# The order of the eighteen products of a step in the expert stage, a different one in each of the four experts

## The chip, the cores and the metric

The kernel runs on one core of a Trainium2 chip. The metric is the device time of one execution in microseconds (us), as a median of several runs. Beside it stands one execution that the hardware profiler recorded.

## The reference, cut to what matters

```python
def _attn_ref(q, k, v, alpha):                 # gated linear attention, state per head
    for t in range(S):
        state = alpha[:, :, t, :, None] * state + np.einsum('bhd,bhe->bhde', k[:, :, t], v[:, :, t])
        y[:, :, t] = np.einsum('bhd,bhde->bhe', q[:, :, t], state)

def _moe_ref(x, w1, w2, w3, w_out):
    a = x @ w1
    b = x @ w2
    h = a * b @ w3
    return h @ w_out

def _moe2_ref(x, domain_probs, w1, w2):        # N 3072 tokens, D 384, E 4 experts, F 1024
    p = domain_probs / (domain_probs.sum(-1, keepdims=True) + 1e-09)
    for e in range(E):
        h = np.maximum(x @ w1[e], 0.0)
        out += p[:, e:e + 1] * (h @ w2[e])
```

The three run one after the other. The change lies in the last one, the four experts.

## The kernel before

Up to about 414 us the kernel computes the attention and the bilinear layer (`up1`, `down1`, products of 384 columns, three split terms each through `split_product`, lines 1061 to 1063). From there on TensorE works on the experts. Tokens are on the columns: 3072 tokens are six tiles of 512, taken two at a time in a round, so three rounds for each expert. F is eight blocks of 128 rows. A step is one block of one tile; a round has sixteen steps (`STEPS2`), steps 0 to 7 on its first tile (u = 0) and 8 to 15 on its second (u = 1).

A step has two halves of nine matrix products each. Every number is split into a high and a low part, so each product of matrices takes three terms (high by high, high by low, low by high), over three blocks of 128 (`KT`).
- U (up, `up2_product`, line 1220): x1 times the expert's first weights, nine products of 128x512 that add up in one PSUM bank, `bank[s % 2]`.
- D (down, `down2_product`, line 1337): h times the expert's second weights. Products 0 to 2 add into a first bank, 3 to 5 into a second, 6 to 8 into a third (`SUM_BANKS[u]`, banks 5, 6, 7 for u = 0, the first two of which the profile calls score_banks, and 2, 3, 4 for u = 1).

`step2(e, m, s, ahead)` waits until the low part of h of step s is ready (`h_lo_ready`), and then issues the nine D of step s and the nine U of step s + 2 in turns: D, U, D, U, and so on. The U of step s + 2 end with a signal (`up_done`), on which h of that step is made on the other engines while TensorE works on step s + 1. In expert 0 this is `h_high` on ScalarE and `h_low` on VectorE. In experts 1 to 3 it is a chain of three: VectorE applies the ReLU and the gate (`scaled_low`, line 1030, out of PSUM into `h_scaled`), ScalarE makes the high part (`scaled_high`, line 726), VectorE the low part (line 1033). After the last step of a tile VectorE adds the three sums to `total` (`add`, lines 1019 to 1023), for which it waits on `down_done`. The last two steps of the last expert have nothing ahead, so they are nine D each. Two of the three rounds of an expert run in a hardware loop, the third is written out.

What makes some U products different is two sets at the top of the file, which `up2_product` looks up by expert, step and product number:

```python
BY_TURNS = {(e, s, i): run for e, run in enumerate((4, 2, 8)) for s, i in ((1, 0), (FT + 1, 4))}
IN_HALVES = {(EXPERTS - 1, s, i) for s, i in ((1, 1), (FT + 1, 4))}
```

A product in `BY_TURNS` computes the same sum in another order of its 512 columns: it takes a run of 4 (2, 8) columns from the first half, then as many from the second half, and so on, in what it reads and in what it writes. A product in `IN_HALVES` is issued as two instructions of 256 columns. Each of these stands twice in every round: at a product of step 1 and of step 9. The text below calls both of them odd products. Expert 0 has odd products with runs of 4, expert 1 of 2, expert 2 of 8, expert 3 the halves. Before the experts' loop, `up2(0, 0, 0)` and `up2(0, 0, 1)` issue nine U each with no D between them, the second with an odd product in front.

Of the kernel before, what the change touches and what calls it, by code (L numbers as in the profile page):

```python
# [26 lines left out]
ALU = mybir.AluOpType  # L27
ACT = mybir.ActivationFunctionType
# [3 lines left out]
BATCH, HEADS, SEQ, D = 4, 8, 768, 48  # L32
# [10 lines left out]
DM, FF, EXPERTS = 384, 1024, 4  # L43
KT, FT = DM // P, FF // P
# [9 lines left out]
TILE2 = 512  # L54
TILES2 = TOKENS // TILE2
STEPS2 = 2 * FT
ROUNDS = TILES2 // 2
# [6 lines left out]
BEGUN_BY_ACT = 2  # L64
FOLD_BANKS = [0, 1, 2, 3, 4, 0, 1, 2]
SUM_BANKS = [[5, 6, 7], [2, 3, 4]]
BY_TURNS = {(e, s, i): run for e, run in enumerate((4, 2, 8)) for s, i in ((1, 0), (FT + 1, 4))}
IN_HALVES = {(EXPERTS - 1, s, i) for s, i in ((1, 1), (FT + 1, 4))}
TERMS = 3
WARM = 6  # L70
CONSTANTS = 7
# [17 lines left out]
def gated_attention_experts(nc, akq, v, akq_long, v_columns, w3T, w_out, wsets, probs, out):  # L89
# [5 lines left out]
    with ExitStack() as ctx:  # L95
        def sb(name, shape, dt=F32, where=ctx):
            return where.enter_context(nc.sbuf_tensor(name, shape, dt))

        def sem(name):
            return ctx.enter_context(nc.semaphore(name))  # L100

        bank = [ctx.enter_context(nc.psum_tensor(f"bank{i}", [P, 512], F32)) for i in range(5)]
# [11 lines left out]
        h_hi = sb("h_hi", [P, 2, TILE2], F32R)  # L114
        h_lo = sb("h_lo", [P, 2, TILE2], F32R)
# [52 lines left out]
        we_raw, we_hi, we_lo, x1_hi, x1_lo = [None, None], [None, None], [None, None], [None, None], [None, None]  # L168
# [18 lines left out]
        gate_rows = [sb(f"gate_rows{i}", [P, TOKENS]) for i in range(2)]  # L187
        h_scaled = sb("h_scaled", [P, 2, TILE2])
# [83 lines left out]
        h_scaled_ready = sem("h_scaled_ready")  # L272
        h_hi_ready = sem("h_hi_ready")
        h_lo_ready = sem("h_lo_ready")
# [36 lines left out]
        def chunk_beside(b, s, last_batch):  # L311
            t, i = divmod(s, FT)
            if i >= 2 * CHUNKS1 or (t == 1 and last_batch):
                return None
            return (b, CHUNKS1 + i // 2) if t == 0 else (b + 1, i // 2)

        def chunk_behind(b, c, count=1):

            n = CHUNKS * b + c + count
            return divmod(n, CHUNKS) if n < BATCH * CHUNKS else None  # L320
# [175 lines left out]
        def _(pool):  # L496
# [30 lines left out]
            def bilinear(b, beside=True, last_batch=False):  # L527
                for s in range(STEPS1):
                    chunk = chunk_beside(b, s, last_batch) if beside else None
                    if chunk and s % 2 and chunk_behind(*chunk, 2):  # L530
                        scale_queries(*chunk_behind(*chunk, 2))
                    if s + 1 < STEPS1 or (beside and not last_batch):
                        g_low(b, s + 1)
                    if last_batch and beside and FT <= s < FT + PIECES // 2:
                        pieces_low(1, s - FT)
                    if last_batch and beside and s == FLAG_STEP:
                        pool.wait_ge(flag_ready, 2)
                        flag = pool.value_load(regular[:, :], min_val=0, max_val=1)
                return flag if last_batch and beside else None
# [20 lines left out]
        def _(act):  # L560
# [161 lines left out]
                h_high(0, 0)  # L722

            def scaled_high(e, m, s):
                act.wait_ge(h_scaled_ready, STEPS2 * ((e - 1) * ROUNDS + m) + s + 1)
                act.activation(h_hi[:, s % 2, :], h_scaled[:, s % 2, :], ACT.Copy).then_inc(h_hi_ready, 1)  # L726

            def step_high(e, m, s):
                if e == 0:
# [21 lines left out]
        def _(dve):  # L751
# [234 lines left out]
            with dve.If(is_regular == 0):  # L986
                dve.sem_inc(redo_value_free, 1)
                dve.sem_inc(redo_y_ready, 1)
                with dve.Fori(0, BATCH) as b:
# [13 lines left out]
                    for c in range(CHUNKS):  # L1003
                        dve.wait_ge(redo_turned, CHUNKS * b + c + 1)
                        t, i = divmod(c, CHUNKS1)
# [18 lines left out]

            def scaled_low(e, m, s):
                n = e * ROUNDS + m
                at = bass.ds((2 * m + s // FT) * TILE2, TILE2)
                dve.wait_ge(gate_rows_loaded[e % 2], 16 * (e // 2 + 1))
                dve.wait_ge(up_done, STEPS2 * n + s + 1)
                dve.scalar_tensor_tensor(out=h_scaled[:, s % 2, :], in0=bank[s % 2][:, :], scalar=0.0, in1=gate_rows[e % 2][:, at],  # L1030
                                         op0=ALU.max, op1=ALU.mult).then_inc(h_scaled_ready, 1)
                dve.wait_ge(h_hi_ready, STEPS2 * n + s + 1)
                dve.tensor_tensor(h_lo[:, s % 2, :], h_scaled[:, s % 2, :], h_hi[:, s % 2, :], ALU.subtract).then_inc(h_lo_ready, 1)  # L1033

            def step_low(e, m, s):
                if e == 0:
# [21 lines left out]
        def _(pe):  # L1058
            def split_product(dst, left, right, first, last):

                pe.matmul(dst, left[0], right[0], start=first, stop=False)  # L1061
                pe.matmul(dst, left[0], right[1], start=False, stop=False)  # L1062
                return pe.matmul(dst, left[1], right[0], start=False, stop=last)  # L1063
# [138 lines left out]
            def up2_waits(e, m, s):  # L1202
                u, f = divmod(s, FT)
                if f == 0:
                    pe.wait_ge(x1_loaded[u], 32 * (e * ROUNDS + m + 1))
                    if u == 0 and isinstance(m, int) and m == 0:
                        pe.wait_ge(piece_lo, PIECES * (e + 2))

            def up2_product(e, s, i):

                u, f = divmod(s, FT)
                k, term = divmod(i, TERMS)
                cols = slice(k * FF + f * P, k * FF + (f + 1) * P)
                parts = [(bank[s % 2][:, :], (x1_lo if term == 1 else x1_hi)[u][:, k, :])]
                if (e, s, i) in BY_TURNS:
                    parts = [tuple(a.rearrange("p (h a r) -> p a h r", h=2, r=BY_TURNS[e, s, i]) for a in part) for part in parts]
                if (e, s, i) in IN_HALVES:
                    parts = [tuple(a[:, half:half + TILE2 // 2] for a in parts[0]) for half in (0, TILE2 // 2)]
                for dst, moving in parts:
                    mm = pe.matmul(dst, (we_hi if term < 2 else we_lo)[e % 2][:, cols], moving, start=(i == 0), stop=(i == KT * TERMS - 1))  # L1220
                if i == KT * TERMS - 1:
                    mm.then_inc(up_done, 1)

# [35 lines left out]
            for k in range(FT):  # L1259
# [5 lines left out]
                for f in range(FOLD_FIRST):  # L1265
                    if (k, f) == (0, 1):
                        pe.wait_ge(w3_loaded[0], 16)
                    cols = slice(f * P, (f + 1) * P)
                    if k < SPLIT_FROM:
                        mm = pe.matmul(bank[FOLD_BANKS[f]][:, 0:DM], w3_sb[:, k, cols], wo_sb[:, k, :], start=(k == 0), stop=False)  # L1270
                    else:
                        i = k - SPLIT_FROM
                        mm = split_product(bank[FOLD_BANKS[f]][:, 0:DM], (w3_hi[:, i, cols], w3_lo[:, k, cols]),
                                           (wo_hi[:, i, :], wo_lo[:, i, :]), False, k == FT - 1)
# [7 lines left out]
            for n in range((FT - FOLD_FIRST) * FT):  # L1282
                f, k = FOLD_FIRST + n // FT, n % FT
# [4 lines left out]
                mm = pe.matmul(bank[FOLD_BANKS[f]][:, 0:DM], w3_sb[:, k, f * P:(f + 1) * P], wo_sb[:, k, :], start=(k == 0), stop=(k == FT - 1))  # L1288
# [14 lines left out]
            with nc.body("redo_products", valid_engines=[pe.engine]):  # L1303
                with pe.Fori(0, BATCH) as b:
                    with pe.Fori(0, REDO_ROWS) as i:
                        pe.wait_ge(redo_product_ready, REDO_ROWS * b + i + 1)
                        for c in range(CHUNKS):
                            mm = pe.matmul(bank[5][:, 2 * c:2 * c + 2], redo_product[:, c * CHUNK:(c + 1) * CHUNK], head_sum[:, :],
                                           start=True, stop=True)
                        mm.then_inc(redo_summed, 1)  # L1310
                    for c in range(CHUNKS):
# [3 lines left out]
                        for k in range(KT):  # L1315
                            mm = pe.transpose(bank[7][:, k * P:(k + 1) * P], y_sb[:, k * P:(k + 1) * P], identity[:, :])
# [11 lines left out]
            def down2_product(e, m, s, i):  # L1328

                u, f = divmod(s, FT)  # L1330
                part, term = divmod(i, TERMS)
                if term == 0 and f == 0:
                    if e == 0 and u == 1 and part == 0:
                        pe.wait_ge(x1_lo_ready, X1_LOW_AHEAD + KT * TILES1 * BATCH)
                    pe.wait_ge(added, KT * (e * TILES2 + 2 * m + u) + part + 1)
                cols = slice(KT * FF + f * DM + part * P, KT * FF + f * DM + (part + 1) * P)
                mm = pe.matmul(bank[SUM_BANKS[u][part]][:, :], (we_hi if term < 2 else we_lo)[e % 2][:, cols], (h_lo if term == 1 else h_hi)[:, s % 2, :],  # L1337
                               start=(f == 0 and term == 0), stop=(f == FT - 1 and term == TERMS - 1))
                if f == FT - 1 and term == TERMS - 1:
                    mm.then_inc(down_done, 1)  # L1340

            def step2(e, m, s, ahead):

                pe.wait_ge(h_lo_ready, STEPS2 * (e * ROUNDS + m) + s + 1)
                if ahead:
                    up2_waits(*ahead)
                for i in range(KT * TERMS):
                    down2_product(e, m, s, i)
                    if ahead:
                        up2_product(ahead[0], ahead[2], i)  # L1350

            def round2(e, m, following):

# [69 lines left out]
```

## Time and profile before

| | us |
|---|---|
| median of 3 runs | 1217.36 (1217.21 to 1217.63) |
| the profiled execution | 1217.92 |
| its span, first to last instruction | 1216.2 |
| TensorE matmul busy, of the span | 1210.0 (99%) |
| TensorE weight load busy | 1039.6 (85%) |
| VectorE busy | 549.2 (45%) |
| ScalarE busy | 287.1 (24%) |
| GpSimd busy | 161.2 (13%) |

The span is 1.7 us shorter than the time of the same execution. A matmul of 512 columns is shown with a length of about 0.39 us, but the next one starts 0.23 us after it: they overlap. The length of one therefore says little; what counts is the distance from one start to the next, called pitch below. The timeline gives starts to 0.01 us, so a pitch is read over many products. A view of stretches counts in "(x...)" also the product that is still running at the start of the stretch; where a stretch begins at the start of a product, the number of pitches in it is one less than that count.

### The profile page before, as it was taken

What the parts mean: (1) busy time and instruction counts of PE and PEld (TensorE: products, weight loads), DVE (VectorE), ACT (ScalarE), POOL (GpSimd) and SP (SyncE); (2) the same over time, 40 slices, a digit from 0 to 9 for tenths busy, and PEclk for the clock granted to TensorE, in tenths of its full rate; (3) what the DMA queues carried; (4) which work ended last, traced back from release to release, by engine and by line L of the source; (5) the groups of instructions that cost most, each with busy time, mean ns of one, the idle gap of its engine ahead of it and who ended that gap; (6) DMA issues with size and microseconds to landing.
All of it is one profiled execution on the core that took longest, in us unless ns stands there. A gap on an engine that the chain in (4) does not pass through costs nothing.

```text
span 1216.2 us, 17647 instructions
## 1 busy us (share of the span) xinstructions
PE 1210.0 (99%) x7170; PEld 1039.6 (85%) x7170; DVE 549.2 (45%) x1006; ACT 287.1 (24%) x526; POOL 161.2 (13%) x147
## 2 busy tenths in 40 slices
PE   9999999999999999999999999999999999999998
PEld 8799999999999988888888888888888888888887
DVE  6997586686651122122233433333343343443433
ACT  3443333333333311111111121121121111111111
POOL 1132222222223400000000000000000000000000
PEclk9999999999999999999999999999999999999999
DMA  9744544544515361101151111114101111222201
GB/s 282 212 122 113 136 130 106 140 126 98 136 47 188 105 259 52 36 19 49 52 207 53 52 52 52 52 63 197 36 19 49 52 52 52 78 78 78 78 7 46
DMA packets 89782, 114.34 MB, mean 94 GB/s; under 512 B 39152, under 2 KB 57968, under 8 KB 88688
## 3 DMA queue, kind: packets, MB, share of 16 engines
q1 hardware_dynamic: 89424, 112.97, 29.5%
q8 instruction: 49, 0.80, 0.3%
q10 hardware_dynamic: 288, 0.39, 0.1%
q14 instruction: 21, 0.17, 0.0%
HBM read 92.59 MB, written 18.40 MB: 91 GB/s over the span
## 4 chain that ended last, share of the span: by engine, by line
PE 98%; DVE 1%; DMA 1%; ACT 0%; SPq 0%; issue 0%; DVEq 0%; ACTq 0%
PE bank L1220 33%; PE bank L1337 22%; PE score_banks L1337 11%; PE bank L1061 9%; PE bank L1063 9%; PE bank L1062 9%; PE bank L1102 2%; PE bank L1288 1%; PE score_banks L1123 1%; PE bank L1112 1%; PE score_banks L1086 1%; DMA wo_sb<-w_out 1%; DVE total L1023 0%; PE bank L1070 0%; DVE w_lo L918 0%; DVE suffix L762 0%
## 5 line engine op out<-in xcount | busy, mean ns | idle before, releaser
L1220 PE MATMUL bank<-x_lo,we_hi 128*128 128x512 f32 x582 | 226.4, 391 | 0.0
L1220 PE MATMUL bank<-x_hi,we_hi 128*128 128x512 f32 x576 | 226.3, 393 | 0.0
L1220 PE MATMUL bank<-x_hi,we_lo 128*128 128x512 f32 x576 | 225.9, 392 | 0.0
L1030 DVE SCALAR_TENSOR_TENSOR h_scaled<-bank,gate_rows 128x512 f32<-128x512 f32 x144 | 99.4, 690 | 253.9 <-PE bank L1220 253.8
L726 ACT ACTIVATE h_hi<-h_scaled 128x512 fp32r<-128x512 f32 x144 | 91.0, 632 | 494.3 <-DVE h_scaled L1030 494.3
L1337 PE MATMUL bank<-h_hi,we_hi 128*128 128x512 f32 x384 | 150.9, 393 | 0.2 <-DVE h_lo L1033 0.2
L1337 PE MATMUL bank<-h_lo,we_hi 128*128 128x512 f32 x384 | 150.8, 393 | 0.0
L1337 PE MATMUL bank<-h_hi,we_lo 128*128 128x512 f32 x384 | 150.7, 392 | 0.0
L1033 DVE TENSOR_TENSOR h_lo<-h_scaled,h_hi 128x512 fp32r<-128x512 f32 x144 | 99.7, 693 | 100.6 <-ACT h_hi L726 100.6
L513 POOL TENSOR_TENSOR we_lo<-we_raw,we_hi (+1 forms) x48 | 60.9, 1292 | 545.2 <-ACT we_hi L574 545.2
L1220 PEld LDWEIGHTS bank<-x_lo,we_hi 128*128 128x128 f32 x582 | 109.3, 188 | 24.8
L1220 PEld LDWEIGHTS bank<-x_hi,we_lo 128*128 128x128 f32 x576 | 108.2, 188 | 24.5
L1220 PEld LDWEIGHTS bank<-x_hi,we_hi 128*128 128x128 f32 x576 | 108.1, 188 | 24.2
L1061 PE MATMUL bank<-x,wb_hi 128*128 128x384 f32 x384 | 128.6, 335 | 0.0
L1063 PE MATMUL bank<-x,wb_lo 128*128 128x384 f32 x384 | 128.4, 334 | 0.0
L1062 PE MATMUL bank<-x,wb_hi 128*128 128x384 f32 x384 | 128.3, 334 | 0.0
L843 DVE SCALAR_TENSOR_TENSOR h_lo<-bank,h_hi 128x512 fp32r<-128x512 f32 x48 | 33.2, 692 | 146.8 <-ACT h_hi L613 146.5
L524 POOL TENSOR_TENSOR g_lo<-g_sb,g_hi 128x384 fp32r<-128x384 f32 x64 | 66.3, 1036 | 221.2 <-ACT g_hi L603 221.1
L1337 PEld LDWEIGHTS bank<-h_hi,we_hi 128*128 128x128 f32 x384 | 72.2, 188 | 16.9 <-DVE h_lo L1033 0.6
L1337 PEld LDWEIGHTS bank<-h_lo,we_hi 128*128 128x128 f32 x384 | 72.2, 188 | 16.3
L1337 PEld LDWEIGHTS bank<-h_hi,we_lo 128*128 128x128 f32 x384 | 72.2, 188 | 16.2
L833 DVE TENSOR_TENSOR g_sb<-a_sb,bank 128x384 f32<-128x384 f32 x64 | 35.3, 552 | 110.8 <-PE bank L1063 110.8
(103 smaller groups left out, 1657.5 us busy)
## 6 DMA issues: line engine op xcount, KB each, us to landing
x_hi<-x_hi_spill SPq DMA_DIRECT2D x24, 768.0 KB, 4.9
x_lo<-x_lo_spill SPq DMA_DIRECT2D x24, 768.0 KB, 6.4
we_raw<-wset SPq DMA_DIRECT2D x4, 3072.0 KB, 10.6
inputs<-akq SPq DMA_DIRECT2D x24, 448.0 KB, 5.0
values<-v_rows SPq DMA_DIRECT2D x24, 256.0 KB, 3.5
gate_rows<-gate_spill SPq DMA_DIRECT2D x4, 1536.0 KB, 13.7
inputs<-akq SPq DMA_DIRECT2D x24, 224.0 KB, 3.3
x_hi_spill<-x_hi_out SPq DMA_DIRECT2D x8, 576.0 KB, 4.2
```

Of the source, the lines that this page charges most:

```text
L513: pool.tensor_tensor(set_lo(n)[:, at], set_raw(n)[:, at], set_hi(n)[:, at], ALU.subtract).then_inc(piece_lo, 1)
L524: pool.tensor_tensor(g_lo[:, s % 2, :], g_sb[:, s % 2, :], g_hi[:, s % 2, :], ALU.subtract).then_inc(g_lo_ready, 1)
L726: act.activation(h_hi[:, s % 2, :], h_scaled[:, s % 2, :], ACT.Copy).then_inc(h_hi_ready, 1)
L833: dve.tensor_tensor(g_sb[:, s % 2, :], a_sb[:, s % 2, :], bank[1][:, 0:TILE1], ALU.mult).then_inc(g_ready, 1)
L843: dve.scalar_tensor_tensor(out=h_lo[:, s % 2, :], in0=bank[s % 2][:, :], scalar=0.0, in1=h_hi[:, s % 2, :], op0=ALU.max, op1=ALU.subtract) ...
L1030: dve.scalar_tensor_tensor(out=h_scaled[:, s % 2, :], in0=bank[s % 2][:, :], scalar=0.0, in1=gate_rows[e % 2][:, at], op0=ALU.max, op1=ALU ...
L1033: dve.tensor_tensor(h_lo[:, s % 2, :], h_scaled[:, s % 2, :], h_hi[:, s % 2, :], ALU.subtract).then_inc(h_lo_ready, 1)
L1061: pe.matmul(dst, left[0], right[0], start=first, stop=False)
L1062: pe.matmul(dst, left[0], right[1], start=False, stop=False)
L1063: return pe.matmul(dst, left[1], right[0], start=False, stop=last)
L1220: mm = pe.matmul(dst, (we_hi if term < 2 else we_lo)[e % 2][:, cols], moving, start=(i == 0), stop=(i == KT * TERMS - 1))
L1337: mm = pe.matmul(bank[SUM_BANKS[u][part]][:, :], (we_hi if term < 2 else we_lo)[e % 2][:, cols], (h_lo if term == 1 else h_hi)[:, s % 2, : ...
```

## The change

The U and D of a step are issued in an order that the expert's number picks from `ORDERS`: expert 0 in turns as before, expert 1 three D and three U, three times, expert 2 two and two (the last pair in turns), expert 3 nine D and then nine U. Each order begins with a D and ends with a U. `IN_HALVES` is gone, and `BY_TURNS` has the same entries for all experts: product 4 of steps 3 and 9, with runs of 4. In the very last step of the kernel, h is made in two halves of 256 columns on VectorE and ScalarE.

```diff
-BY_TURNS = {(e, s, i): run for e, run in enumerate((4, 2, 8)) for s, i in ((1, 0), (FT + 1, 4))}
-IN_HALVES = {(EXPERTS - 1, s, i) for s, i in ((1, 1), (FT + 1, 4))}
+ORDERS = [9 * "DU", 3 * ("DDD" + "UUU"), 4 * "DDUU" + "DU", 9 * "D" + 9 * "U"]
+BY_TURNS = {(e, s, 4): 4 for e in range(EXPERTS) for s in (3, FT + 1)}
...
+        def h_parts(e, m, s):
+            last = isinstance(m, int) and (e, m, s) == (EXPERTS - 1, ROUNDS - 1, STEPS2 - 1)
+            return [slice(0, TILE2 // 2), slice(TILE2 // 2, TILE2)] if last else [slice(0, TILE2)]
...
             def scaled_high(e, m, s):
-                act.wait_ge(h_scaled_ready, STEPS2 * ((e - 1) * ROUNDS + m) + s + 1)
-                act.activation(h_hi[:, s % 2, :], h_scaled[:, s % 2, :], ACT.Copy).then_inc(h_hi_ready, 1)
+                for i, at in enumerate(h_parts(e, m, s)):
+                    act.wait_ge(h_scaled_ready, STEPS2 * ((e - 1) * ROUNDS + m) + s + 1 + i)
+                    act.activation(h_hi[:, s % 2, at], h_scaled[:, s % 2, at], ACT.Copy).then_inc(h_hi_ready, 1)
...
             def scaled_low(e, m, s):
                 n = e * ROUNDS + m
-                at = bass.ds((2 * m + s // FT) * TILE2, TILE2)
                 dve.wait_ge(gate_rows_loaded[e % 2], 16 * (e // 2 + 1))
                 dve.wait_ge(up_done, STEPS2 * n + s + 1)
-                dve.scalar_tensor_tensor(out=h_scaled[:, s % 2, :], in0=bank[s % 2][:, :], scalar=0.0, in1=gate_rows[e % 2][:, at],
-                                         op0=ALU.max, op1=ALU.mult).then_inc(h_scaled_ready, 1)
-                dve.wait_ge(h_hi_ready, STEPS2 * n + s + 1)
-                dve.tensor_tensor(h_lo[:, s % 2, :], h_scaled[:, s % 2, :], h_hi[:, s % 2, :], ALU.subtract).then_inc(h_lo_ready, 1)
+                for part in h_parts(e, m, s):
+                    at = bass.ds((2 * m + s // FT) * TILE2 + part.start, part.stop - part.start)
+                    dve.scalar_tensor_tensor(out=h_scaled[:, s % 2, part], in0=bank[s % 2][:, part], scalar=0.0, in1=gate_rows[e % 2][:, at],
+                                             op0=ALU.max, op1=ALU.mult).then_inc(h_scaled_ready, 1)
+                for i, part in enumerate(h_parts(e, m, s)):
+                    dve.wait_ge(h_hi_ready, STEPS2 * n + s + 1 + i)
+                    dve.tensor_tensor(h_lo[:, s % 2, part], h_scaled[:, s % 2, part], h_hi[:, s % 2, part], ALU.subtract).then_inc(h_lo_ready, 1)
...
-                parts = [(bank[s % 2][:, :], (x1_lo if term == 1 else x1_hi)[u][:, k, :])]
+                dst, moving = bank[s % 2][:, :], (x1_lo if term == 1 else x1_hi)[u][:, k, :]
                 if (e, s, i) in BY_TURNS:
-                    parts = [tuple(a.rearrange("p (h a r) -> p a h r", h=2, r=BY_TURNS[e, s, i]) for a in part) for part in parts]
-                if (e, s, i) in IN_HALVES:
-                    parts = [tuple(a[:, half:half + TILE2 // 2] for a in parts[0]) for half in (0, TILE2 // 2)]
-                for dst, moving in parts:
-                    mm = pe.matmul(dst, (we_hi if term < 2 else we_lo)[e % 2][:, cols], moving, start=(i == 0), stop=(i == KT * TERMS - 1))
+                    dst, moving = [a.rearrange("p (h a r) -> p a h r", h=2, r=BY_TURNS[e, s, i]) for a in (dst, moving)]
+                mm = pe.matmul(dst, (we_hi if term < 2 else we_lo)[e % 2][:, cols], moving, start=(i == 0), stop=(i == KT * TERMS - 1))
...
             def step2(e, m, s, ahead):
 
-                pe.wait_ge(h_lo_ready, STEPS2 * (e * ROUNDS + m) + s + 1)
+                pe.wait_ge(h_lo_ready, STEPS2 * (e * ROUNDS + m) + s + len(h_parts(e, m, s)))
                 if ahead:
                     up2_waits(*ahead)
-                for i in range(KT * TERMS):
-                    down2_product(e, m, s, i)
-                    if ahead:
-                        up2_product(ahead[0], ahead[2], i)
+                ups = downs = 0
+                for product in ORDERS[e]:
+                    if product == "D":
+                        down2_product(e, m, s, downs)
+                        downs += 1
+                    elif ahead:
+                        up2_product(ahead[0], ahead[2], ups)
+                        ups += 1
```

## Rows read from the trace of the kernel before

**Rows 1.** The page's TensorE clock in 40 slices, and TensorE's waits from 420 us on.
```profile
PEclk9999999999999999999999999999999999999999
...
engine line waited for: us in total, times, longest us
PE bank L1337 <- DVE h_lo L1033: 0.2, 1, 0.2
```
**Rows 2.** Stretches: TensorE busy (x products), clock, DMA share, GB/s; expert 0 to 3.
```profile
420.32:615.54 195.22, 195.22 (x847) 1.00 0.23 83
615.54:814.90 199.36, 199.36 (x865) 1.00 0.20 72
814.90:1014.16 199.26, 199.26 (x867) 1.00 0.20 72
1014.16:1208.17 194.01, 194.01 (x850) 1.00 0.16 56
```
**Rows 3.** The same view, two stretches of expert 0 with no odd product inside.
```profile
421.49:451.35 29.86, 29.86 (x129) 1.00 0.78 297
485.24:517.90 32.66, 32.66 (x143) 1.00 0.14 46
```
**Rows 4.** Timeline: two odd products of expert 0, and where the 0.230 pitch begins.
```profile
451.58 0.42 PE L1220 MATMUL bank<-x_lo,we_hi 128*128 128x512 f32 x1
...
453.23 0.39 PE L1337 MATMUL bank<-h_hi,we_lo 128*128 128x512 f32 x1
...
482.90 0.41 PE L1220 MATMUL bank<-x_hi,we_hi 128*128 128x512 f32 x1
...
485.01 0.39 PE L1337 MATMUL bank<-h_hi,we_lo 128*128 128x512 f32 x1
```
**Rows 5.** Timeline: first and last of nine U (odd product in front of the second nine).
```profile
414.12 0.39 PE L1220 MATMUL bank<-x_hi,we_hi 128*128 128x512 f32 x1
...
415.98 0.40 PE L1220 MATMUL bank<-x_hi,we_lo 128*128 128x512 f32 x1
...
418.02 0.40 PE L1220 MATMUL bank<-x_lo,we_hi 128*128 128x512 f32 x1
...
419.65 0.40 PE L1220 MATMUL bank<-x_hi,we_lo 128*128 128x512 f32 x1
```
**Rows 6.** Timeline: fifteen products of 384 columns, three or nine in a bank.
```profile
300.13 0.33 PE L1063 MATMUL bank<-g_hi,wp_lo 128*128 128x384 f32 x1
...
302.56 0.33 PE L1062 MATMUL bank<-x,wb_hi 128*128 128x384 f32 x1
```
**Rows 7.** Timeline: the last two steps, nine D each, with the chain between.
```profile
1208.17 0.39 PE L1337 MATMUL bank<-h_hi,we_hi 128*128 128x512 f32 x1
...
1208.44 0.69 DVE L1030 SCALAR_TENSOR_TENSOR h_scaled<-bank,gate_rows 128x512 f32<-128x512 f32 x1 [2.06 <-PE bank L1220]
...
1209.16 0.63 ACT L726 ACTIVATE h_hi<-h_scaled 128x512 fp32r<-128x512 f32 x1 [3.51 <-DVE h_scaled L1030]
...
1209.83 0.69 DVE L1033 TENSOR_TENSOR h_lo<-h_scaled,h_hi 128x512 fp32r<-128x512 f32 x1 [0.70 <-ACT h_hi L726]
...
1210.01 0.39 PE L1337 MATMUL bank<-h_hi,we_lo 128*128 128x512 f32 x1
...
1210.57 0.50 PE L1337 MATMUL bank<-h_hi,we_hi 128*128 128x512 f32 x1 [0.18 <-DVE h_lo L1033]
...
1210.91 0.40 PE L1337 MATMUL bank<-h_lo,we_hi 128*128 128x512 f32 x1
...
1212.55 0.39 PE L1337 MATMUL bank<-h_hi,we_lo 128*128 128x512 f32 x1
```
**Rows 8.** Groups by shape: the nearest shorter operations of VectorE and ScalarE.
```profile
L798 DVE TENSOR_TENSOR scores<-score_banks,causal 64x256 f32<-64x256 f32 x24 | 10.3, 428 | 0.3
...
L603 ACT ACTIVATE g_hi<-g_sb 128x384 fp32r<-128x384 f32 x64 | 33.6, 526 | 122.0 <-DVE g_sb L833 122.0
```
**Rows 9.** Timeline of VectorE in a usual step of expert 3: one step's two operations.
```profile
1030.25 0.69 DVE L1030 SCALAR_TENSOR_TENSOR h_scaled<-bank,gate_rows 128x512 f32<-128x512 f32 x1 [2.06 <-PE bank L1220]
1031.64 0.69 DVE L1033 TENSOR_TENSOR h_lo<-h_scaled,h_hi 128x512 fp32r<-128x512 f32 x1 [0.70 <-ACT h_hi L726]
```

## The prediction

> **What bounds the kernel now.** I read the clock first, then TensorE's waits, then stretches of the expert stage, then single products. The granted clock is full in all forty slices, which is the 2.4 GHz level, and from 420 us on TensorE waits once, for 0.2 us, just before the last nine products [rows 1]. So the expert stage is one unbroken stream of products, and its time is their number times the pitch. No other engine and no DMA is on the path until the end.
>
> The pitch is not one number. In the first stretch of expert 0 it is 29.86 / 128 = 0.2333 us, in a later one 32.66 / 142 = 0.2300 us [rows 3]. Both are D and U in turns, with the same shapes, banks and weights. What lies between them is one odd product at 451.58: seven pitches later, at 453.23, the short pitch begins and stays [rows 4]. The stream thus has at least two settled rhythms, 0.2300 and 0.2333, and the start of the stage finds the long one. The reader is to see in the four experts' stretches that the short one then holds to the end: the excess over 0.2300 times the number of 512-column products is 195.22 - 846 x 0.2300 = 0.64 us in expert 0, 199.36 - 864 x 0.2300 = 0.64 in expert 1, 199.26 - 866 x 0.2300 = 0.08 in expert 2, and 194.01 - 843 x 0.2300 = 0.12 in expert 3, whose 849 pitches hold six products in two halves [rows 2]. The sum is 1.48 us.
>
> **The odd products.** Where the stream is already in the short rhythm, an odd product with runs of 4 costs 2.11 us over nine pitches instead of 2.07, so 0.04 us [rows 4]. Before, 0.43 us of expert 0's excess is its long rhythm up to 451.58 (about 134 pitches by 0.0033), the rest its odd products. After, expert 0 has the first odd product with a D between its neighbours at product 4 of step 3, which is issued beside step 1, some 27 pitches from the start instead of 134. That leaves 27 x 0.0033 = 0.09 us of long rhythm, 0.04 for the product, and 5 x 0.04 = 0.20 for the other five, so 0.33 us instead of 0.64. If experts 1 to 3 stayed in the short rhythm, they would pay 18 x 0.04 = 0.72 us instead of 0.64 + 0.08 + 0.12 = 0.84. This part alone brings 0.31 + 0.12 = 0.43 us.
>
> **The last step in halves.** Before, VectorE starts the last h at 1208.44, ScalarE at 1209.16, VectorE again at 1209.83, and TensorE goes on at 1210.57, 0.56 us after the product before it, where 0.23 was due [rows 7]. The chain is 0.69 + 0.63 + 0.69 plus gaps of about 0.03. In halves, a VectorE operation of 256 columns is nearest to the row of 0.43 us; for ScalarE 384 columns take 0.53 and 512 take 0.63, so 256 about 0.42, an estimate by the difference [rows 7, 8]. The first half of the high part starts 0.46 us into the chain, the second ends 0.46 + 0.42 + 0.03 + 0.42 = 1.33, and the second low part ends at about 1.33 + 0.03 + 0.43 = 1.79, since VectorE is done with its first low part by then. Before it was 2.08. That is 0.3 us less of the 0.33 us stall. The longer first pitch behind the wait (0.34 instead of 0.23 [rows 7]) stays if TensorE still arrives first; bounds 0 (each half costs as much as a whole) and 0.44 (stall and longer pitch both gone), taken 0.30. Behind it, the last nine D, the adds and the store are as before.
>
> **The orders, as far as waits go.** Every order begins with D and ends with U, so `up_done` of the step ahead comes at the end of the same eighteen products as before. The chain on it starts at 1030.25 and ends at 1032.33 [rows 9], while TensorE has 18 x 0.23 = 4.14 us of the step between to do. About 2 us of cover stand behind it, and no order takes from that. `down_done` of the third sum comes earlier in the three new orders (in nine and nine after 9 of 18 products instead of 17), so the adds end earlier. In nine and nine the three waits on `added` are three products apart instead of six, but they ask for adds a whole tile back, 8 steps or 33 us. Nothing is queued behind them on TensorE that was not due anyway. Loads of x1 hang on `up_done` as before. I cost this at nothing; if the cover were gone, each late step would show as a wait of TensorE on h_lo.
>
> **The orders, as far as the pitch goes.** This decides. The new orders put products of the same kind behind each other: 12 of 18 pitches in expert 1, 8 of 18 in expert 2, 16 of 18 in expert 3. With 48 steps (46 with something ahead in expert 3) that is 576 + 384 + 736 = 1696 pitches, half from U to U, half from D to D, 848 each. Rows for such pitches are few. U to U: (415.98 - 414.12) / 8 = 0.2325 and (419.65 - 418.02) / 7 = 0.2329, both long, though the first nine came out of a stream without any wait and the second had an odd product in front [rows 5]. D to D: (1210.01 - 1208.17) / 8 = 0.2300 out of the short rhythm, and (1212.55 - 1210.91) / 7 = 0.2343 after the wait [rows 7]. Against an effect of the kind speaks the stream of 384 columns, where products follow in one bank three or nine at a time: (302.56 - 300.13) / 14 = 0.1736 with no sign of a second rhythm [rows 6]. I take 0.0025 us for each U to U and the middle of the D rows, (0 + 0.0043) / 2, cut to 0.0015 since the first of the two is the nearer case (it runs out of the short rhythm, as these will). The sum is 848 x 0.0025 + 848 x 0.0015 = 2.12 + 1.27 = 3.39 us. The pitches between kinds stay at 0.2300. A stream that is not in the short rhythm pays less for an odd product: seven pitches from 451.58 take 1.65 us instead of 7 x 0.2333 = 1.63, so 0.02 and not 0.04 [rows 4]; with 18 of them about 0.4 us less.
>
> The sum against the profiled execution: 1217.92 - 0.43 - 0.30 + 3.39 - 0.36 = 1220.2. Against the median of the runs, which is 0.56 us under the profiled execution, it is 1217.36 + 2.30 = 1219.7. That is the forecast.
>
> A rule against all this. At one column in a cycle of the 2.4 GHz level, 512 columns would take 0.2133 us, and the short rhythm has 0.2300 [rows 3], so 0.0167 us a product are something else; if that something were the change of bank, the new orders would save it. The Trainium skill, TensorE: Matmul & The Clock Gate, section "Back-to-back issue gap", gives N / 2.4 + 2.5 ns, 215.8 ns for 512 columns, and the same page, "A second HAM failure mode", says that cycling through PSUM banks makes TensorE idle for moments. By these the pitch could come down towards 0.216; the trace doesn't agree where it has products in one bank [rows 5, 6].
>
> **The rivals.**
> 1. The rhythm does not care for the kind, and the odd products keep all four experts at 0.2300. For it: 384-column products [rows 6], and that every odd product of experts 1 to 3 was followed by the short rhythm again, whatever the banks [rows 2]. Against: both rows of U to U. Time 1217.36 - 0.43 - 0.30 = 1216.6. Chance 0.30.
> 2. The orders of experts 1 to 3 throw the whole stream into the long rhythm, changes of kind too, slower than before: 2592 pitches x 0.0033 = 8.6 us, less 0.84 us of odd products no longer paid over the short rhythm, less 0.31 of expert 0, less 0.30 at the end: 1224.5. It decides from the point where an odd product within a run fails to bring the short rhythm back, as it did in front of the second nine U [rows 5]. The other row for it is the start of expert 0 in the long rhythm [rows 3]. Chance 0.15.
> 3. D to D runs faster than 0.2300. The first eight average 0.2300 with the change of rhythm among them, so later ones may be shorter. If 848 pitches gained 0.0033, the distance of the two known rhythms, it were 2.8 us: 1213.8. Chance 0.08.
> 4. The 0.0167 us over one column a cycle is the cost of changing banks, and a product in the bank of the one before saves it. U to U always is one, D to D two times in three or more: about 848 + 570 = 1418 pitches by 0.0167, 24 us, so 1193. Against it stand the U to U rows, all in one bank, at 0.2325 [rows 5]. Chance 0.02.
> 5. The change doesn't do what it says, because TensorE is held up elsewhere (a queue of waits that fills at nine and nine): nothing in the rows for it, perhaps +1 us in expert 3 alone. Chance 0.03.
>
> **How the numbers follow.** The forecast, same-kind runs partly out of the short rhythm, has 0.42. Its own range is 1217.5 (D to D free, U to U half of what is taken) to 1222 (all same-kind pitches at 0.2333 and some of the others). Rivals 1 and 2 are taken into the range: 1214.5 to 1224.8, which leaves out rivals 3 and 4 and little else. Within 0.2% of before (2.4 us, about what a measurement of this kernel can tell from no change) means 1214.9 to 1219.8. Rival 1, rival 5 and about half of the forecast lie in it: 0.30 + 0.03 + 0.21 = 0.54. Slower: 0.21 + 0.15 = 0.36. Faster: rivals 3 and 4, 0.10.
>
> **What would show it.** In stretches of the changed kernel, one for each expert: expert 0 at 0.2304 a pitch, expert 2 about 0.231, expert 1 about 0.2315, expert 3 about 0.232. All four near 0.2303 is rival 1; experts 1 to 3 at 0.2333 is rival 2; one of them under 0.2300 is rival 3. The short rhythm in expert 0 should begin near 428 us, not 453. TensorE's wait before the last nine products should be gone or under 0.1 us, and nowhere else should there be a wait on h_lo. The prediction is wrong in its ground if the experts differ by a wait and not by the pitch.

## The result and the profile after

The changed kernel takes 1219.93 us (median of 12 runs, 1219.13 to 1221.48), the kernel before 1217.28 (12 runs, 1216.86 to 1217.89). The ratio is 1.002 with a 95% interval of 1.0013 to 1.0028: 2.65 us slower. The forecast was 1219.7, and the range holds the time. The difference is 0.22% of the time, just over the 0.2% that the prediction drew as the line between the same and slower, and the forecast lay just under it; the prediction had given the likelier side, 0.54, to "the same". The terms behind the forecast were partly wrong in ways that cancel, and the reason for the pitches was not the one given. Both come out below.

| | before | after |
|---|---|---|
| median of the runs, us | 1217.28 | 1219.93 |
| the profiled execution | 1217.92 | 1219.17 |
| its span | 1216.2 | 1217.4 |
| first D of the experts to the last, us | 419.98 to 1212.55 | 418.87 to 1213.82 |
| that stage | 792.57 | 794.95 |

The profiled executions differ by 1.25 us only, because this one reached the experts 1.11 us earlier, in a part of which the change touches one odd product, worth 0.02 us. The stage itself is 2.38 us longer, which is the difference of the medians within their spread.

The view of stretches, one for each expert from its first D to the next expert's first, in the changed kernel (columns: TensorE busy (x products), granted clock, DMA share, GB/s). It answers to [rows 2]:

```profile
418.87:618.03 199.16, 199.16 (x866) 1.00 0.24 85
618.03:817.60 199.57, 199.57 (x866) 1.00 0.20 71
817.60:1018.82 201.22, 201.22 (x866) 1.00 0.20 71
1018.82:1209.88 191.06, 191.06 (x830) 1.00 0.15 54
```

48 steps of 18 products are 864 pitches (46 steps and 828 in the last row), so the mean pitches are 0.2305, 0.2310, 0.2329 and 0.2307 us. The count of the view is a little higher, since it takes in the products that overlap the ends. The clock is full throughout, and TensorE's waits from 420 us on, the view of [rows 1], are an empty list now:

```profile
engine line waited for: us in total, times, longest us
```

So no wait came in. What differs is how far the products stand apart. In expert 3 (nine and nine) the timeline has first a stretch of U, then one of D:

```profile
1145.72 0.40 PE L1224 MATMUL bank<-x_lo,we_hi 128*128 128x512 f32 x1
...
1147.59 0.40 PE L1341 MATMUL bank<-h_hi,we_hi 128*128 128x512 f32 x1
1147.82 0.39 PE L1341 MATMUL bank<-h_lo,we_hi 128*128 128x512 f32 x1
...
1149.63 0.40 PE L1224 MATMUL bank<-x_hi,we_hi 128*128 128x512 f32 x1
```

Eight pitches of U take 1147.59 - 1145.72 = 1.87 us, 0.2338 each. Eight pitches behind the first D take 1149.63 - 1147.82 = 1.81 us, 0.2263 each, give or take the 0.01 us of the view. In a step away from odd products the nine pitches that begin with a U average 0.2334 us. Of the nine that begin with a D, the first takes 0.2325 and the others 0.2267. The mean of 0.2334 and 0.2267 is 0.2300, the short rhythm of the kernel in turns, and the longer first D makes the step 4.147 us against 4.140.

In expert 2 (two and two) the same step takes longer:

```profile
870.69 0.39 PE L1341 MATMUL bank<-h_hi,we_hi 128*128 128x512 f32 x1
...
874.88 0.39 PE L1341 MATMUL bank<-h_hi,we_hi 128*128 128x512 f32 x1
```

One step is 874.88 - 870.69 = 4.19 us, 0.05 more than in turns, and nearly every step of that expert is so. Of the 2.38 us, this order alone brings 201.22 - 864 x 0.2300 = 2.50 us.

### The profile page after: what moved, and what is told of

Read it like the earlier page. It is cut to its first block, busy times and chain, and to the rows that moved or that the text cites. A ratio compares the mean times of both kernels' runs of the same rounds, so it can differ in the third digit from the quotient of the medians.

```text
span 1217.4 us, 17638 instructions
## 1 busy us (share of the span) xinstructions
PE 1212.0 (100%) x7164; PEld 1039.2 (85%) x7164; DVE 549.5 (45%) x1008; ACT 286.9 (24%) x527; POOL 161.0 (13%) x147
## 4 chain that ended last, share of the span: by engine, by line
PE 99%; DVE 0%; issue 0%; ACT 0%; DVEq 0%
PE bank L1224 33%; PE bank L1341 22%; PE score_banks L1341 11%; PE bank L1068 9%; PE bank L1070 9%; PE bank L1069 9%; PE bank L1109 2%; PE bank L1292 1%; PE score_banks L1130 1%; PE bank L1119 1%; PE score_banks L1093 1%; PE bank L1274 1%; PE bank L1262 0%; DVE total L1028 0%; PE bank L1077 0%
## 5 line engine op out<-in xcount | busy, mean ns | idle before, releaser
L1036 DVE SCALAR_TENSOR_TENSOR h_scaled<-bank,gate_rows 128x512 f32<-128x512 f32 (+1 forms) x145 | 99.6, 687 | 263.0 <-PE bank L1224 262.7
L731 ACT ACTIVATE h_hi<-h_scaled 128x512 fp32r<-128x512 f32 (+1 forms) x145 | 91.1, 629 | 497.1 <-DVE h_scaled L1036 497.1
L1040 DVE TENSOR_TENSOR h_lo<-h_scaled,h_hi 128x512 fp32r<-128x512 f32 (+1 forms) x145 | 99.8, 689 | 100.0 <-ACT h_hi L731 100.0
```

The lines of the kernel that those rows point to most:

```text
L731: act.activation(h_hi[:, s % 2, at], h_scaled[:, s % 2, at], ACT.Copy).then_inc(h_hi_ready, 1)
L1036: dve.scalar_tensor_tensor(out=h_scaled[:, s % 2, part], in0=bank[s % 2][:, part], scalar=0.0, in1=gate_rows[e % 2][:, at], op0=ALU.max, o ...
L1040: dve.tensor_tensor(h_lo[:, s % 2, part], h_scaled[:, s % 2, part], h_hi[:, s % 2, part], ALU.subtract).then_inc(h_lo_ready, 1)
```

## The experiments

Each kernel is the changed one with the edit shown or told.

**e1: all experts in turns.** Is it the orders at all?

```diff
-ORDERS = [9 * "DU", 3 * ("DDD" + "UUU"), 4 * "DDUU" + "DU", 9 * "D" + 9 * "U"]
+ORDERS = [9 * "DU"] * EXPERTS
```

> The changed kernel with all four experts in turns (D, U, D, U), the odd products and the last step as in the changed kernel. Theory (the new orders cost the time, through the pitch): every expert at 0.2300 us a pitch plus six odd products of 0.04 us, expert stage about 792.0 us instead of 794.95, time about 1216.6, so 0.7 under the kernel before. Rival (something else of the change costs the time, the odd products or the halves at the end): experts 1 to 3 stay above 0.2305 and the time near 1219.9.

1216.77 us, ratio to the kernel before 0.9995 (0.9985 to 1.0005). The stretches:

```profile
419.82:618.98 199.16, 199.16 (x866) 1.00 0.24 85
618.98:817.94 198.96, 198.96 (x866) 1.00 0.20 72
817.94:1016.90 198.96, 198.96 (x866) 1.00 0.20 72
1016.90:1207.58 190.68, 190.68 (x830) 1.00 0.15 54
```

198.96 is 864 x 0.2300 + 6 x 0.04, to 0.01 us. The orders of experts 1 to 3 cost 0.61 + 2.26 + 0.38 = 3.25 us, and without them the rest of the change is 0.5 us quicker than before in the medians, which the interval doesn't tell from nothing.

**e2: no odd products.** What do they do in each order?

```diff
-BY_TURNS = {(e, s, 4): 4 for e in range(EXPERTS) for s in (3, FT + 1)}
+BY_TURNS = {}
```

> The changed kernel without any odd product. Theory (an order has several rhythms and an odd product only moves the stream from one to another): expert 0 keeps the long rhythm from its start, 0.2333 us a pitch, 4.20 us a step instead of 4.14, about 2.5 us more in that expert; expert 1 stays in one of its two rhythms (4.14 or 4.16 us a step) to the end; expert 3, whose runs of nine settle by themselves, stays at 4.147 us a step. Rival (the order alone sets the pitch): no expert changes by more than the odd products' own 0.04 us each, and expert 0 is at 0.2300.

1222.70 us in the one run, a span of 1220.9.

```profile
419.94:621.65 201.71, 201.71 (x866) 1.00 0.23 84
621.65:821.33 199.68, 199.68 (x865) 1.00 0.20 71
821.33:1022.59 201.26, 201.26 (x865) 1.00 0.20 71
1022.59:1213.37 190.78, 190.78 (x830) 1.00 0.15 54
```

Expert 0 stays in the long rhythm to its end, 201.71 / 864 = 0.2335, 2.55 us over the changed kernel. Three and three stays at 4.160 us a step in all its steps. In the changed kernel it is at 4.160 in most and at 4.140 in four steps behind each odd product of step 3; the one of step 9 ends that. Two and two is at 4.193 with and without odd products, and nine and nine at 4.147. So the first theory holds: in turns and three and three have two settled rhythms each. In turns an odd product moved the stream from the long one to the short one; in three and three it did so in either direction. Of two and two and of nine and nine, one rhythm each was seen. Without odd products experts 1 to 3 take 199.68, 201.26 and 190.78 us, with them 199.57, 201.22 and 191.06: in these orders the 18 odd products cost 0.13 us in all.

**e4: the D ordered by term.** Does the PSUM bank matter, or that products share weights?

```diff
-                part, term = divmod(i, TERMS)
+                term, part = divmod(i, KT)
```

(in `down2_product`)

> The changed kernel with the nine D of a step ordered by term first and bank second, so that every D goes to another bank than the D before it and shares no weights with it. Theory B (bank): the pitch within the nine D of expert 3, 0.2267 us with bank changes at every third product, falls further or at least changes, and the D to D pitches of experts 1 and 2 change. Theory A (placement of the moving operand): all D to D pitches stay as they were, 4.147 us a step in expert 3.

1220.91 us in the one run. Every D now goes to another bank than the one before it, and shares no weights with it. The stretches have the same lengths as those of the changed kernel, all four:

```profile
419.69:618.85 199.16, 199.16 (x866) 1.00 0.24 85
618.85:818.42 199.57, 199.57 (x866) 1.00 0.20 71
818.42:1019.64 201.22, 201.22 (x866) 1.00 0.20 71
1019.64:1210.70 191.06, 191.06 (x830) 1.00 0.15 54
```

That leaves neither the bank nor shared weights as a reason for the pitch of the D. What still tells D from U is, before all, the tile that they read.

**e3: x1 moved by 32 bytes.** The tiles' order and sizes (each rounded up to 32 bytes) give where each starts in its partition. In the changed kernel, and in the one before, h_hi starts at byte 3552, x1 at 11968 and the experts' weights at 174560 and 54752. Modulo 128 these are 96, 64, 96 and 96: h lies as the weights do, x1 32 bytes off.

```diff
+        sb("x1_pad", [P, 8])
         for slot in range(2):
             x1_hi[slot] = sb(f"x1_{slot}_hi", [P, KT, TILE2], F32R)
             x1_lo[slot] = sb(f"x1_{slot}_lo", [P, KT, TILE2], F32R)
-        sb("attention_rest", [P, ATTENTION_REST])
+        sb("attention_rest", [P, ATTENTION_REST - 8])
```

> The changed kernel with the four x1 tiles placed 32 bytes further in each partition, nothing else. In the changed kernel a U behind a U takes 0.2333 us and a D behind a D 0.2267. Theory A (it goes by where the moving operand lies against a 64-byte line: h lies 32 bytes off the alignment of x1): U to U falls to 0.2267 us, expert 3 goes from 4.147 to about 4.08 us a step, expert 0 may fall to 4.08 too, in all up to 10 us less. Theory B (it goes by the PSUM bank: U stays nine products in one bank, D three): U to U stays at 0.2333 and no expert changes.

1204.96 us, ratio to the kernel before 0.9901 (0.9884 to 0.9917). This is 15 us under the changed kernel, by moving four tiles by 32 bytes.

```profile
419.36:615.56 196.20, 196.20 (x866) 1.00 0.24 87
615.56:811.64 196.08, 196.08 (x866) 1.00 0.20 73
811.64:1007.72 196.08, 196.08 (x866) 1.00 0.20 73
1007.72:1195.64 187.92, 187.92 (x830) 1.00 0.16 55
```

The reader is to see that four different orders now take the same time: 196.08 = 864 x 0.22667 + 6 x 0.04, so 4.08 us a step whatever the order, with 4.12 at the odd products. Theory B falls. Of theory A this shows that the place of x1 counts, but not yet that a 64-byte line is what it is measured against. The expectation left it open whether expert 0 would get there; it does, 0.12 us later than the others for its first pitches.

**e5, e6, e9, e10 and e7: is it x1's own place, or its place against the weights?** e5 moves h by 32 bytes (a pad of 8 columns before `h_hi`, one behind `h_lo`), and with the two pads all tiles behind h by 64. e6 moves the experts' weights by 32, and with them the tiles behind them (`total`, the gate rows, `h_scaled`). e9 moves all so that all start at 0 modulo 128 (e3 with the first pad of e5). e10 moves x1 by 96 (a pad of 24). e7 starts each x1 tile 48 bytes into a tile made 64 bytes longer, so the four don't lie alike.

> The changed kernel with h_hi and h_lo placed 32 bytes further, so that h starts on a 64-byte line of its partition, as x1 does in the changed kernel, while the expert weights stay 32 bytes off one. Theory A1 (a moving operand that starts on a 64-byte line is the slow one): D is now like U, all four experts go to the long rhythm, 0.2333 us a pitch, 4.20 us a step in every order, time about 1228. Theory A2 (what counts is only that h and x1 lie alike): all steps 4.08 us and a time near 1205, as with x1 moved.

> The changed kernel with the experts' weights (and what lies behind them: total, gate rows, h_scaled) placed 32 bytes further, so that they start on a 64-byte line; x1 starts on one and h lies 32 bytes off, both as in the changed kernel. Theory A1 (it is the moving operand's own place): steps as in the changed kernel, 4.140, 4.160, 4.193 and 4.147 us. Theory A3 (it is the place of the moving operand relative to that of the weights): the kinds change roles, U to U 0.2267 us and D to D 0.2333; expert 3 stays near 4.147 us a step but with the short pitch in its U.

> The changed kernel with x1 placed 48 bytes past a 64-byte line (16 past the place that was quick in e3, which was 32 past). If any start off a 64-byte line is quick: all steps 4.08 us and a time near 1205. If 32-byte alignment is needed as well: U to U at 0.2333 us or more and a time of 1220 or more.

> The changed kernel with h, x1 and the experts' weights all starting on a 64-byte line (h and the weights moved by 32 bytes, x1 by 64, all now on a 128-byte line). Theory A3 (the place of the moving operand relative to the weights counts, and it is the same for both kinds here): all steps 4.08 us with 4.12 at the odd products, time about 1205, as in e3. Theory A4 (both operands must start off a 64-byte line, as in e3): all steps 4.20 us, time about 1227, as in e5.

> The changed kernel with x1 moved by 96 bytes instead of the 32 of e3, so 64 bytes past the place that was quick; h and the weights stay. Theory A3 with a period of 128 bytes (x1 is now 64 bytes off the weights, as it was in e6, where U stayed slow): U to U at 0.2333 us or near, time 1218 or more. Theory A4, or A3 with a period of 64 bytes: all steps 4.08 us, time about 1205.

Places are bytes modulo 128; pitches are the means of the four stretches, worked out as above. The times are of one run each for e5, e6, e7, e9 and e10.

| | h | x1 | weights | time, us | pitch of experts 0 to 3, us |
|---|---|---|---|---|---|
| changed kernel | 96 | 64 | 96 | 1219.93 | 0.2305, 0.2310, 0.2329, 0.2307 |
| e3 | 96 | 96 | 96 | 1204.96 | 0.2271, 0.2269, 0.2269, 0.2270 |
| e5 | 0 | 0 | 32 | 1227.22 | 0.2335, 0.2333, 0.2333, 0.2334 |
| e6 | 96 | 64 | 0 | 1225.57 | 0.2330, 0.2313, 0.2320, 0.2333 |
| e7 | 96 | 112 and 48 | 96 | 1220.27 | 0.2316, 0.2312, 0.2320, 0.2311 |
| e9 | 0 | 0 | 0 | 1205.06 | 0.2271, 0.2269, 0.2269, 0.2270 |
| e10 | 96 | 32 | 96 | 1222.74 | 0.2318, 0.2328, 0.2310, 0.2305 |

The stretch of expert 3 in e5:

```profile
1024.63:1217.91 193.28, 193.28 (x829) 1.00 0.15 53
```

The same stretch in e6:

```profile
1023.22:1216.36 193.14, 193.14 (x830) 1.00 0.15 53
```

And in e9:

```profile
1007.95:1195.87 187.92, 187.92 (x829) 1.00 0.15 55
```

e5: with h and x1 alike but 32 bytes off the weights, all orders sit at 0.2333, and D is as slow as U was. That h and x1 lie alike is not enough (A2 falls). e9: all at 0, all quick, and the same as e3 to 0.01 us a stretch. A4, that both must start off a 64-byte line, falls with that. The clearest pair is e5 against e9: h starts at byte 3584 and x1 at 12032 in both, only the weights and what lies behind them have moved by 32 bytes, and the pitch is 0.2333 us in one and 0.2267 in the other. So it isn't the moving operand's own place (A1 falls).

e6 came out as neither A1 nor A3 had it. With the weights moved, the stretch of nine and nine is 193.14 / 828 = 0.2333: D is slow (D to D 0.2327), which A3 expected, but U is too (U to U 0.2340), though x1 is then 64 bytes off the weights. So equal places modulo 64 don't do. e10 says the same, with x1 moved on by 64 from where it was quick and 1222.74 us. But e10 also shows that the pitch of a D does not go by its own operands alone. In its expert 3 neither h nor the weights have moved, and still:

```profile
1147.31 0.39 PE L1342 MATMUL bank<-h_lo,we_hi 128*128 128x512 f32 x1
...
1149.16 0.40 PE L1225 MATMUL bank<-x_hi,we_hi 128*128 128x512 f32 x1
```

These are the same eight pitches as behind the first D above, 1.85 us here and 1.81 there, 0.2313 each against 0.2263. Where x1 lies reaches into the run of nine D behind its U. The D of e6 could have been slowed that way as well; the pair e5 and e9 doesn't hang on it.

e7 lies between its two cases: 1220.27 us, no order at 4.08 us a step, and U to U at 0.2310 to 0.2323 us in experts 1 to 3. It has something that the other runs can't show. Its first pair of x1 tiles (read by the U of steps 0 to 7) and its second pair (steps 8 to 15) start at the same bytes modulo 128, but 128 apart modulo 256: high parts at 240 and 112, low parts at 48 and 176. Expert 2, three steps with U of the first pair, then five with U of the second, none with an odd product:

```profile
831.65:844.11 12.46, 12.46 (x55) 1.00 0.04 14
856.67:877.63 20.96, 20.96 (x91) 1.00 0.00 1
```

That is 4.153 us a step and 4.192. U run two steps ahead, so those of the second pair begin beside the D of step 6. That is where the pace changes, and it changes back at step 14, in every round. In the changed kernel, whose pairs lie alike modulo 256 as well, expert 2 has 4.193 in both. So the place modulo 128 doesn't settle the pace.

The Trainium skill, TensorE: Matmul & The Clock Gate, section "Step-by-step: what each phase is for", gives TensorE two separate ports into SBUF, so that loading the next weights takes no read bandwidth from the running matmul. From that one would not expect the places of the two operands to matter to each other; e5 and e9 do not agree, at 0.2333 and 0.2267 us.

What stands is A3 (the place of the moving operand against that of the weights) with a period of more than 128 bytes. In e3 and e9 the pitch is 0.2267 us in every order, and in both h, x1 and the weights start at the same byte modulo 256 (224 in e3, 0 in e9). Modulo 512 they don't: x1 is 256 off in both. A distance of exactly 128 bytes for all tiles was not run. e6 and e10 came to the experts at 421.6 us, the others by 419.9; that part of their times is not of the experts.

**e8: what beats both.** x1 moved as in e3, all experts in turns, no odd products.

> x1 moved by 32 bytes as in e3, all experts in turns, and no odd products; the halves at the end stay. Theory (with all operands placed alike there is one rhythm only, which needs no odd product to be found): 4.08 us in every step from the start, 24 odd products by 0.04 us less than e3, time about 1204.0. Rival (the start of the stage falls into a long rhythm again without an odd product): expert 0 at 4.10 us a step or more, time above 1206.

1204.32 us, ratio to the kernel before 0.9894 (0.9878 to 0.9911).

```profile
419.59:615.59 196.00, 196.00 (x866) 1.00 0.24 87
615.59:811.43 195.84, 195.84 (x866) 1.00 0.20 73
...
1007.27:1194.95 187.68, 187.68 (x830) 1.00 0.16 55
```

195.84 is 864 x 0.22667. The stream is in the quick rhythm from its second step on, and nothing has to bring it there. Against e3 the experts lose the 24 x 0.04 = 0.96 us of the odd products: 776.28 to 775.36 us over the four stretches, 0.92.

## Why the prediction came out right, and where it didn't

**The bound.** Right. The stage is one stream of products, and after the change it has no wait at all. The cover put at about 2 us behind h held in every order.

**Odd products and expert 0.** Right to 0.01 us. The short rhythm begins behind the odd product at 425.28:

```profile
425.28 0.42 PE L1224 MATMUL bank<-x_lo,we_hi 128*128 128x512 f32 x1
...
427.16 0.39 PE L1224 MATMUL bank<-x_hi,we_lo 128*128 128x512 f32 x1
```

Expert 0 has 199.16 - 864 x 0.2300 = 0.44 us over the short rhythm, of which 0.11 is its first pitch behind the wait, which the stretch of [rows 2] left out. The rest is the 0.33 that was forecast. e1 confirms 0.04 us for each of the later ones. In experts 1 to 3 of the changed kernel the odd products cost 0.13 us in all against e2, where 0.36 was forecast, because they also moved the rhythm.

**The last step in halves.** Forecast 0.30 us, measured 0.39, inside the bounds of 0 and 0.44. The rows of after that answer to [rows 7]:

```profile
1210.15 0.76 DVE L1036 SCALAR_TENSOR_TENSOR h_scaled<-bank,gate_rows 128x256 f32<-128x256 f32 x2 [2.06 <-PE bank L1224]
...
1210.61 0.75 ACT L731 ACTIVATE h_hi<-h_scaled 128x256 fp32r<-128x256 f32 x2 [3.25 <-DVE h_scaled L1036]
...
1211.06 0.76 DVE L1040 TENSOR_TENSOR h_lo<-h_scaled,h_hi 128x256 fp32r<-128x256 f32 x2 [0.15 <-ACT h_hi L731]
...
1211.70 0.39 PE L1341 MATMUL bank<-h_hi,we_lo 128*128 128x512 f32 x1
1211.92 0.44 PE L1341 MATMUL bank<-h_hi,we_hi 128*128 128x512 f32 x1
1212.21 0.39 PE L1341 MATMUL bank<-h_lo,we_hi 128*128 128x512 f32 x1
```

The chain from 1210.15 to 1211.82 is 1.67 us instead of 2.08; a pair of halves takes 0.76 us on VectorE, where twice 0.43 was put. The stall before the last nine D is gone (1211.70 to 1211.92), and of the longer pitch behind it 0.29 is left where 0.34 was. Together 0.56 + 0.34 = 0.90 us before and 0.51 after.

**The orders' pitches.** The sum was near, 3.39 + 0.36 us forecast for experts 1 to 3 against 199.57 - 198.72 = 0.85, 2.50 and 191.06 - 190.44 = 0.62 measured, in all 3.97. That was luck, since its terms were not right. By kind of pitch, over 0.2300 each, from the starts of all products of the trace, odd ones and what follows them included: U to U was taken at 0.0025 and measured 0.0032 to 0.0039, 3.1 us instead of 2.12. D to D was taken at +0.0015 and measured -0.0020 in nine and nine, -0.0010 in three and three, +0.0025 in two and two: -0.5 us instead of 1.27. The step that failed outright is "the pitches between kinds stay at 0.2300". In two and two a D behind a U takes 0.2357, 1.4 us over 240 of them, and the pitches between kinds together cost 1.4 us that stood in no term. Hence the order of the experts was wrong: forecast 0.2315, 0.231 and 0.232, measured 0.2310, 0.2329 and 0.2307. The order with the most neighbours of one kind is not the dearest.

**The two rows of D to D.** The forecast read [rows 7] as 0.2300 and 0.2343 and took less than the middle. Neither is the settled D to D of the changed kernel's nine and nine, 0.2267, and both look like streams that had not settled: eight pitches out of the rhythm in turns, and seven behind a wait. Rival 3 had the mechanism (D to D at 0.2267), without that of U going the other way beside it.

**The rivals.** Rival 1 falls with e1: with the orders undone, 3.25 us go. Rival 2 is what e5 does in all orders, 4.20 us a step and 1227.22 us, when D is out of place too; in the changed kernel D isn't. Rival 4 falls with e4 and with every row of U to U, and with it what the prediction drew from the Trainium skill, TensorE: Matmul & The Clock Gate, sections "Back-to-back issue gap" and "A second HAM failure mode": more products in one bank brought no pitch near 0.216. Rival 5 falls with the empty list of waits.

**Right for a reason that was not the real one.** The prediction held that neighbours of one kind leave a rhythm. The runs show that kind has no part in it but for where its tile lies: with x1 placed as the weights are, the four orders take 4.08 us a step alike (196.08 us for 48 steps, 187.92 for the 46 of expert 3), the 0.12 of expert 0's start aside.

## What to carry to other kernels

When a stream of matmuls has no wait and its pitch is still some per cent over that of another stream with the same shapes, compare where its operands start. Here 32 bytes in the place of one operand were worth 1.2% of the changed kernel, and 1.0% of the one before, while the orders and the odd products moved between 1216.77 and 1222.70 us and the change of bank did nothing. Test it with a pad of a few columns before working on the order.

## What the runs showed of the hardware that was not expected

- Products of 128x512 with all operands in SBUF alike modulo 256 bytes follow each other after 0.2267 us, at full granted clock; with moving operand and weights 32 bytes apart, after 0.2333 us (e3, e9 against e5).
- With the operands of D alike and those of U 32 bytes apart, the stream has rhythms of its own: 0.2300 or 0.2333 us in turns, 4.140 or 4.160 us a step in three and three, in two and two only 4.193 was seen. In turns and in three and three it stays in one for hundreds of products (all of e2) until an odd product moves it.
- The pitch of a product goes also by what its neighbours read: with x1 64 bytes off the weights, eight pitches in a run of D take 1.85 us instead of 1.81, their own operands unmoved (e10).
- Equal places modulo 128 are not equal in effect: x1 tiles 128 apart modulo 256 gave steps of 4.153 and 4.192 us in one expert (e7).
- The rhythm is exact. Two executions of different kernels (the changed one and e4) agree in each of four stretches of 200 us to 0.01 us.
- Open: what in the reading of operands makes the 0.0067 us, why e6, e7 and e10 lie between, and what a distance of exactly 128 bytes does. The products of 384 columns stay at about 0.174 us in all kernels, their operands alike modulo 256 in all of them; they were not tried apart.
